# Filter rows loaded in pairs, and weight blocks prepared at other places, in an FFT filter with two MLPs behind it

## The reference

```
def _attn_ref(x, filt_r, filt_i):               # x: (2, 3008, 256)
    X = np.fft.rfft(x, axis=1)
    Y = X * (filt_r + 1j * filt_i)[None, :, :]   # filters: (1505, 256)
    return np.fft.irfft(Y, n=x.shape[1], axis=1).astype(np.float32)

def _moe_ref(x, w_in, w_out):                   # (6016, 256) x (256, 2048) x (2048, 256)
    h = x @ w_in
    return (np.maximum(0.01 * h, h) @ w_out).astype(np.float32)

def _moe2_ref(x, w_in, w_out):
    r = np.maximum(x @ w_in, 0.0)
    return ((r * r) @ w_out).astype(np.float32)
```

## Time and profile before

| | us |
|---|---|
| median of 3 runs | 1119.35 (1119.31 to 1119.74) |
| the profiled execution | 1118.84 |
| its span in the trace | 1116.8 |
| TensorE busy | 1091.4 (98%) |
| DVE / ACT / POOL busy | 770.4 / 564.4 / 298.1 |

### The profile page before, as it was taken

How to read it: one execution, slowest core, us unless ns; L and a number is a source line. 1 busy time by engine, 2 the same in 40 slices (tenths; PEclk the granted TensorE clock), 3 DMA queues, 4 the chain that set the end, 5 groups by cost and what they waited for, 6 DMA issues and landing times.

```text
span 1116.8 us, 14070 instructions
## 1 busy us (share of the span) xinstructions
PE 1091.4 (98%) x5088; PEld 915.0 (82%) x5088; DVE 770.4 (69%) x1181; ACT 564.4 (51%) x979; POOL 298.1 (27%) x291
## 2 busy tenths in 40 slices
PE   8998789999999999999999999999999999999998
PEld 8777668888888888888888888888888888888887
DVE  2996477777676776677666776676666766676665
ACT  3554345555455565555455554454454554554443
POOL 0796523223334234224221021111120120210000
PEclk9999899999999999999999999999999999999999
DMA  9778500011211211211134300000000000000000
GB/s 316 217 248 263 172 1 1 1 36 43 59 41 43 64 50 44 49 50 49 47 125 155 123 1 1 38 1 1 38 1 1 36 1 1 38 1 1 38 1 35
DMA packets 71956, 67.91 MB, mean 61 GB/s; under 512 B 41040, under 2 KB 55760, under 8 KB 71888
## 3 DMA queue, kind: packets, MB, share of 16 engines
q1 hardware_dynamic: 71744, 66.83, 19.2%
q10 hardware_dynamic: 144, 0.20, 0.1%
HBM read 43.02 MB, written 23.99 MB: 60 GB/s over the span
## 4 chain that ended last, share of the span: by engine, by line
PE 93%; POOL 2%; DMA 1%; ACT 1%; DVE 1%; issue 1%; SPq 0%; DVEq 0%
PE PS L867 15%; PE PS L866 15%; PE PS L868 15%; PE PS L874 13%; PE PS L876 13%; PE PS L875 13%; PE PS L789 2%; PE PS L826 2%; PE PS L816 2%; POOL YF L396 1%; PE PS L805 1%; DMA WIF<-in_w1i 1%; PE PS L838 1%; POOL WIL L321 1%; ACT WIH L493 1%
## 5 line engine op out<-in xcount | busy, mean ns | idle before, releaser
L596 ACT ACTIVATE GH<-GF 128x512 fp32r<-128x512 f32 (+1 forms) x384 | 238.6, 622 | 226.0 <-DVE GF L741 116.5
L747 DVE TENSOR_TENSOR GL<-GF,GH 128x512 fp32r<-128x512 f32 (+1 forms) x384 | 260.0, 682 | 109.8 <-ACT GH L596 103.3
L867 PE MATMUL PS<-GL,WOH 128*128 128x512 f32 (+1 forms) x768 | 296.8, 387 | 0.0
L866 PE MATMUL PS<-GH,WOH 128*128 128x512 f32 (+1 forms) x768 | 296.8, 386 | 0.0
L868 PE MATMUL PS<-GH,WOL 128*128 128x512 f32 (+1 forms) x768 | 296.6, 386 | 0.0
L874 PE MATMUL PS<-XH,WIH 128*128 128x512 f32 (+1 forms) x672 | 260.5, 388 | 4.1 <-DVE YL L698 2.4
L876 PE MATMUL PS<-XH,WIL 128*128 128x512 f32 (+1 forms) x672 | 259.3, 386 | 0.0
L715 DVE TENSOR_TENSOR GF<-PS,GF 128x512 f32<-128x512 f32 (+1 forms) x96 | 65.3, 680 | 171.8 <-ACT GF L567 171.8
L868 PEld LDWEIGHTS PS<-GH,WOL 128*128 128x128 f32 x768 | 144.4, 188 | 27.8
L867 PEld LDWEIGHTS PS<-GL,WOH 128*128 128x128 f32 x768 | 144.4, 188 | 27.8
L866 PEld LDWEIGHTS PS<-GH,WOH 128*128 128x128 f32 x768 | 144.3, 188 | 27.7
(11 more groups left out here) (62 smaller groups left out, 1015.4 us busy)
## 6 DMA issues: line engine op xcount, KB each, us to landing
FL<-in_filt SPq DMA_DIRECT2D x32, 224.0 KB, 3.9
zu<-U SPq DMA_DIRECT2D x32, 192.0 KB, 3.5
V<-zu SPq DMA_DIRECT2D x12, 512.0 KB, 6.0
X<-in_x SPq DMA_DIRECT2D x8, 512.0 KB, 8.8
out_y<-YT SPq DMA_DIRECT2D x4, 1024.0 KB, 4.3
wi<-PWH SPq DMA_DIRECT2D x16, 224.0 KB, 2.5
wi<-PWL SPq DMA_DIRECT2D x16, 224.0 KB, 3.1
WIH<-wi SPq DMA_DIRECT2D x8, 448.0 KB, 3.5
```

What stands on the lines that cost most here:

```text
L596: nc.scalar.activation(GH[:, g, 0:width(s)], GF[:, g, 0:width(s)], ACT.Copy).then_inc(g_hi[kind], 1)
L747: nc.vector.tensor_tensor(GL[:, g, 0:w], GF[:, g, 0:w], GH[:, g, 0:w].bitcast(f32), ALU.subtract).then_inc(g_lo[kind], 1)
L866: nc.tensor.matmul(acc, wh, xh, start=first, stop=False)
L867: nc.tensor.matmul(acc, wh, xl, start=False, stop=False)
```

## The change

- Filter rows come two units at a time. FL has four slots of three rows each (was five slots of two). The real filter of each of the two units stays in both halves of the partitions, as L665's product needs it. Of the imaginary filter there is no second copy any more: the first unit's lies in partitions 0 to 47, the second's from 64 on, in one row. Both half products of a unit read it from there.
- Tables and filter rows are loaded by functions of their own, tables six units ahead. A filter slot is free when the products of both of its units are done.
- XF has three buffers. DVE waits for POOL's sum of the unit three before, where it waited for the one two before.
- Weight blocks 0 to 3 are prepared inside the filter stage, in rounds of seven units. Blocks 4 to 6 are loaded right behind the last store, ahead of V1, and rounded behind the YT copies 7, 9 and 11. Block 7 is loaded among the WOF loads and summed, rounded and split in steps 1 to 3 of the MLP.

```
-FSLOTS = 5
+FSLOTS = 4
-    XF = at("XF", [KR, 2, B, 2 * 128], f32, 34 * KB)
-    U = at("U", [K2, USLOTS, 2, B * 128], f32, 38 * KB)
+    XF = at("XF", [KR, 3, B, 2 * 128], f32, 34 * KB)
+    U = at("U", [K2, USLOTS, 2, B * 128], f32, 40 * KB)
-    FL = at("FL", [KR, FSLOTS, 2, 2 * 128], f32, o_x)
+    FL = at("FL", [KR, FSLOTS, 3, 2 * 128], f32, o_x)
-        WI_EARLY = 6
+        WI_UNITS, WI_STEP = 4, 7
...
+            def load_filter(f):
+                if f >= FSLOTS:
+                    sp.wait_ge(prod, 3 * 2 * (f - FSLOTS + 1))
+                sp.dma_start(FL[:, f % FSLOTS, :, :], filt[:, f, :, :]).then_inc(ft_in[f % FSLOTS], 16)
...
             for i in range(UNITS):
-                if i + FSLOTS < UNITS:
-                    load_filter(i + FSLOTS)
+                if i + 6 < PAIRS:
+                    load_table(i + 6)
+                if i % 2 == 0 and i // 2 + FSLOTS < PAIRS:
+                    load_filter(i // 2 + FSLOTS)
                 store_u(i)
-                if i % 5 == 2 and i // 5 + 1 < KU:
-                    load_w1i(i // 5 + 1)
+                if i % WI_STEP == WI_STEP - 1 and i // WI_STEP + 1 < WI_UNITS:
+                    load_w1i(i // WI_STEP + 1)
...
+            for k in range(WI_UNITS, KU - 1):
+                load_w1i(k)
             for g in range(MH // 4):
                 load_v(1, g)
-            load_w1i(KU - 1)
 
             sp.wait_ge(y_ps, CH)
             for k in range(KU):
                 sp.dma_start(WOF[:, k, :], w1o[:, k, :]).then_inc(wo_raw[k], 16)
+                if k == 1:
+                    load_w1i(KU - 1)
...
-            for k in range(2, KU):
-                beside_psum(k)
-                wo_split(k)
-                if k < 4:
-                    x_forms(1, k - 2)
+            for s in range(1, KU):
+                beside_psum(s)
+                if s == 1:
+                    for part in range(2):
+                        wi_sums(KU - 1, part)
                 else:
-                    x_split(1, k - 4)
+                    wo_split(s)
+                if s == 3:
+                    for part in range(3):
+                        wi_split(KU - 1, part)
+                if s in (2, 3):
+                    x_forms(1, s - 2)
+                if s >= 4:
+                    x_split(1, s - 4)
...
-                if i % 5 == 3 and i // 5 < WI_EARLY:
-                    wi_round(i // 5)
+                if i % WI_STEP == 4 and i // WI_STEP < WI_UNITS:
+                    wi_round(i // WI_STEP)
...
-                if c == 5:
-                    wi_round(6)
-                if c == 7:
-                    wi_round(7)
+                if c in (7, 9, 11):
+                    wi_round(WI_UNITS + (c - 7) // 2)
...
+                if s == 2:
+                    wi_round(KU - 1)
...
-                if i >= 2:
-                    dve.wait_ge(yf_sb, i - 1)
                 if i >= 3:
+                    dve.wait_ge(yf_sb, i - 2)
                     dve.wait_ge(u_ps, i - 2)
                 P = PS[0:KR, 2 + i % 2, :].rearrange("p (b d) -> p b d", b=B)
-                fr, fi = (FL[:, i % FSLOTS, c:c + 1, :] for c in range(2))
+                fr = FL[:, f % FSLOTS, i % 2:i % 2 + 1, :]
+                fi = FL[IM * (i % 2):IM * (i % 2) + R, f % FSLOTS, 2:3, :]
```

60 lines of the change are left out of this document (31 added, 29 removed).

## The result

The changed kernel takes 1110.3 us (median of 4 runs, 1108.67 to 1111.18) beside 1119.55 us for the kernel before on the same chip (4 runs, 1119.31 to 1121.67). The ratio is 0.9912, with a 95% interval of 0.9894 to 0.9929: 9.25 us, or 0.9%, faster. The forecast was 1109.2, within 1105.6 to 1113.5. The profiled execution took 1108.67 us, with a span of 1106.9; against the profiled execution of before, 1118.84, that is 10.2 us, the forecast gain. The profiled execution is the fastest of the four, so the medians, 9.25 us apart, are the better measure of the gain.

The account below looks back on a forecast made before the run. The MLPs are bound by untouched matmuls, so only earlier work counts: X forms move from 129.89 to 119.7, 10.2 us, 1.5 of it the filter stage's. 1118.84 - 10.2 = 1108.6, as a median 1109.2, range 1105.6 to 1113.5.

Parts of the forecast that it names:

- The start: Filter stage start: pad MEMSET grows from 0.95 to 1.42 us and unit 0's second product waits, +0.47 us.
- Rounds of seven: Filter stage: POOL needs 13.3 us per seven units against 15.2, so units keep 2.17 us.
- W: Filter stage: POOL's wait for weight blocks 1 to 3 landing after 4.3 us; 1.8 us, bounds 0 and 3.9.
- E: Start of the filter stage's last inverse: forecast 101.6 us against 103.13, 1.5 us gained.
- rival 1: End of filter stage: clock falls to half, contrary to half-busy windows at 140; T' = 120.8, 1110.2 us; chance 20%.
- T': Start of POOL's X forms behind the filter stage: forecast to move from 129.89 to 119.7, 10.2 us gained.
- Block 4's landing: Behind the last store: block 4, issued at E + 2.11, lands in 3.3 us, bounds 2.1 and 5.6.
- Block 7 beside the MLP: MLP steps 1 to 3: POOL's and ACT's work on block 7 costs zero, at most 1 us.
- 2, the worst landings: Filter stage and behind: W = 3.9, last landing 5.6 us; gain only 5.8, 1113.6 us; chance 14%.
- 3, the shortest: Filter stage and behind: W = 0, last landing 2.6 us; gain 12.5, 1106.9 us; chance 18%.
- 4: Filter products reading filter and spectrum on different partitions lengthen; at double time 1131 us, 12 slower; chance 3%.
- 5: MLP start: block 7's 5.3 us of POOL and ACT all stop TensorE; 1114.5 us; chance 5%.

Follow-up runs that it names:

- a3: Changed kernel with XF back to two buffers, VectorE waiting for POOL's sum of the unit two before; 1109.81 us, ratio 0.9895.
- c2: As c1, but with two XF buffers; 1104.67 us, ratio 0.9862.
- b1: Changed kernel with filter rows loaded unit by unit again, imaginary filter twice, 224 KB per unit, five slots; 1111.27 us, ratio 0.9934.
- after: The changed kernel, unaltered, in its first measurement; 1110.3 us, ratio 0.9912 to the kernel before.
- a1: The changed kernel once more, no edit; 1110.96 us, ratio 0.9908.
- a2: Changed kernel with the loads of weight blocks 4 to 6 behind the six V1 loads instead of ahead; 1121.01 us, ratio 0.9996.
- c4: The changed kernel a third time, no edit, on the chip of the c runs; 1111.59 us, ratio 0.9921.
- b2: Changed kernel with the loads of weight blocks 1 to 3 issued one unit earlier; 1108.07 us, ratio 0.9896.
- c3: Changed kernel with block 7 loaded behind block 6 and prepared ahead of the X forms, not in the MLP; 1113.34 us, ratio 0.9939.
- b3: Changed kernel with the first two sequence steps put between the last three inverses of the filter stage; 1109.07 us, ratio 0.9906.
- b4: Changed kernel with rounds of six, blocks 0 to 4 in the stage, loads one unit earlier and b3's gap steps; 1107.02 us, ratio 0.9877.
- c1: b4 with blocks 5 to 7 loaded at units 26, 28, 30 and all prepared before the X forms; 1104.18 us, ratio 0.9860.
- a4: Changed kernel with five-unit rounds, blocks 0 to 5 prepared there, block 6 loaded at unit 27, block 7 in the MLP; 1111.98 us, ratio 0.9922.

## Why the prediction was right

**The time.** 1109.2 was forecast and 1110.3 measured (1110.96 and 1111.59 on two other chips); the profiled executions differ by 10.17 us, where 10.2 was worked out. Point by point:

- **The start:** 0.47 us for the larger MEMSET; measured 0.46 at the inverse of unit 2. The MEMSET itself gave 0.42: from its start to this inverse it takes 9.86 us with three XF buffers, and 9.43 to 9.44 with two (a3, c2). Another 0.13 is new in all of these, before it was 9.31. It is absent in b1 (9.73), so it goes with the paired filter rows and their loading. In the measured 0.46 the earlier start of the MEMSET hides 0.09.
- **Rounds of seven:** units at 2.17 us. That holds (2.17 in the chain).
- **W, POOL's wait for late blocks:** taken as 1.8 us, measured 0.36 in the profiled execution; over the executions of the change and its variants it ranged from nothing to 2.3 (2.94 with the larger filters). The term was mis-sized by the landing of block 1, for which I took 5.6 us from the earlier trace rows and which landed in 4.6 (the 4.58 in the chain above). So E was 100.17, not 101.6. The term took every microsecond that POOL waits as one of E, and that was too much: against 62.71 without late loads, waits of 0.36, 0.92 and 1.09 us (after, a1, a2) moved E - S by 0.08, 0.29 and 0.39. The last unit was taken 0.43 us too short, 3.78 us from the inverse of unit 29 to the last, measured 4.21. In c4 one late block did more than the whole term.
- **The clock:** rival 1's condition came true, with 20% given. The last inverse ran at 1.2 GHz and took 2.02 us instead of 1.10, and the issue of block 4 came at E + 3.02, not E + 2.11. The price was 0.9 us, not 1.1, and it came by another way than the rival's: not by late sequence steps and ACT's round, which was over at 112.05, before POOL's first split at 112.54, but by the store and the load that stand behind the slow inverse. That the median, 1110.3, meets the rival's 1110.2 is chance: the profiled execution with this fall took 1108.67. The row that I leaned on, that at 140, was not the nearer one. With the same two gaps of 1.03 to 1.06 us the clock fell here and in a1, a2, b2 and c3, and stayed in a3, b1 and c4; where it stayed, T' - E is 18.5 to 18.8 us, where it fell 18.9 to 19.4 (after, a1, b2). What decides between them is open. No fall was seen there in b3, b4, c1 and c2, whose gaps are filled.
- **Block 4's landing:** 3.65 us from issue to the first sum, with 3.3 taken between 2.1 and 5.6.
- **Sums and splits:** 5.7 and 7.0 us; measured 5.70 (106.84 to 112.54) and 6.99 (112.54 to 119.53). As forecast, the forms stand directly behind the splits, and ACT's round was over at 112.05, just before POOL wanted it.
- **T':** 119.7 forecast, 119.53 measured. The sum is right within 0.2 us because W (1.4 too large) and clock plus landing (0.9 + 0.35 too small) nearly cancel. This is luck; its parts are only good to about 1.5 us each. The two other profiled executions of the same kernel had T' at 120.16 and 123.62.
- **The path before:** the prediction says that the 6.69 us stall goes and that the rest of the gain is POOL's. It does not say that before, the forms waited for the YT copy (3.65 us) and not for POOL, with the sequence restarted at half clock. Its T' of after is worked out from POOL's line and does not rest on this.
- **Block 7 beside the MLP:** taken as nothing, at most 1 us. TensorE waits 0.5 us for it, and in M - T' no price is seen.

For the last point, the timeline of the changed kernel in the MLP, at its fifth step:

```profile
189.60 0.69 DVE L764 TENSOR_TENSOR GL<-GF,GH 128x512 fp32r<-128x512 f32 x1 [0.70 <-ACT GH L609]
...
191.62 2.40 POOL L399 TENSOR_TENSOR XL<-XT,XH 128x1024 fp32r<-128x1024 f32 x1
...
191.87 3.90 DVE L756 SCALAR_TENSOR_TENSOR GF<-GF 128x512 f32<-128x512 f32 x3
...
195.77 0.50 PE L891 MATMUL PS<-XH,WIH 128*128 128x512 f32 x1 [0.46 <-ACT SN L587]
```

Before, three such DVE operations at the same step took less and TensorE did not wait:

```profile
202.29 3.35 DVE L739 SCALAR_TENSOR_TENSOR GF<-GF 128x512 f32<-128x512 f32 x3
...
205.65 0.50 PE L874 MATMUL PS<-XH,WIH 128*128 128x512 f32 x1
```

POOL's L399 now lies beside DVE's operations for 2.15 us (191.87 to 194.02), before for 1.61 (202.29 to 203.90), and they are longer by 0.55, which is just about the difference. ACT's work, the copy into SN among it, comes late by that, and TensorE waits. That block 7 is what shifts POOL there is shown by c1, c2 and c3, which have it out of the MLP and have no such wait.

**The rivals.** 1 came true in its condition, at 0.9 us, and did not change the outcome. 2, the worst landings, was not seen in the execution shown above, but that of c4, at 1113.35, comes close to its 1113.6, though by one late block and the clock rather than by three late blocks and a landing of 5.6 us at the end. 3, the shortest, was never seen: the first of the loads behind the last store landed in 3.58 us here and in 3.57 at the best of the executions of this kernel, where the rival had 2.6. The Trainium skill (DMA: Bandwidth & Descriptors, Anatomy of one DMA) states the rule that gave that 2.6, an estimate, for transfers issued by GpSimd. These are issued by SP, and the rule is a us short for this one, with only the last store ahead of it on the queue. The shortest landing of all runs, 3.1 us in a4, is above it too. 4 is refuted by the products' lengths, and 5 by TensorE's waits in the MLP.

**What the sum did not tell:** that the two parts do not add up. The filter stage was given 1.5 us and the tail 8.7. With the new stage but the loads behind V1 nothing is gained (a2), and with the stage as slow as before, block 7 in the MLP and no load behind the store, 8.5 us are (a4). The rounds of seven that shorten the stage leave more blocks behind it, so that the two parts can't be had one without the other, and no run has the new stage with the old tail.

## What to carry to other kernels

A wait of TensorE has its length in one place and its price in another: the 6.7 us for an ACT copy were one end of a line, from a load over POOL's sums and ACT's round, that the order of loads on one queue held up. Ask what must be finished before the next stage begins, add it up on its in-order engine from the first landing on, and put the loads in front of others that are not wanted so soon. Issue a load one step earlier than its usual landing time asks for: b2, b4, c1 and c2 did so at no cost that is seen, and none of them waited for a block in the filter stage.

## What the runs showed of the hardware

**The last store.** Executions with nearly equal M (1101.55 in b2, 1101.50 in a3) end 2.1 us apart, and the end lies 4.7 to 7.2 us behind M. The last DMA issue of b2 and of a3:

```profile
1103.03 0.55 SPq L304 DMA_DIRECT2D out_y<-YT  x1
```

```profile
1102.98 2.03 SPq L304 DMA_DIRECT2D out_y<-YT  x1
```

In nine of the fourteen executions the issue took 0.55 us and the span ended 4.7 us behind M; in a2, a3, b3, b4 and c4 it took 0.62 to 2.03 us and the span ended 6.2 to 7.2 us behind. Where the issue itself was short, as in b3, the store landed late. The cause is open. It is why T' and M are the finer yardstick here.

**Landing times.** In the filter stage (from 39 us on) and right behind the last store, ahead of V1, a load of the same 256 KB landed in 3.1 (a4) to 6.25 us (c4), and in different executions of one kernel the same block was in time or 2.26 us late.

**DVE beside POOL.** The remainders YL read two SBUF operands and take 1.79 us and then 2.04 us each, where the like operation L764 above takes 0.69 with POOL idle. YT's copies, which read PSUM, keep 0.69 us beside the same POOL work.

```profile
119.63 0.69 DVE L696 COPY YT<-PS 128x512 f32<-128x512 f32 x1 [1.31 <-PE PS L855]
120.91 1.79 DVE L715 TENSOR_TENSOR YL<-YT,XH 128x512 fp32r<-128x512 f32 x1 [0.59 <-POOL XT L379]
...
123.96 6.12 DVE L715 TENSOR_TENSOR YL<-YT,XH 128x512 fp32r<-128x512 f32 x3 [0.65 <-POOL XT L384]
```

The Trainium skill (SBUF — State Buffer, SBUF: two separate sides) says that a DVE operation with two SBUF inputs and a GpSimd operation hold a shared port pair one at a time, each for its whole instruction. It limits this to a GpSimd operation that reads SBUF, as POOL's sums and splits do. The traces agree in kind: of the DVE operations shown here only those with two SBUF inputs grow. They don't show the size: three operations of 0.69 us, beside POOL's L399 for 2.15 us, grew to 3.90, by 1.83.
